# Linear attention ahead of two expert layers: 24 tiles pipelined two ahead, prefix sums in rounded parts, inputs in long rows

## Chip, cores and metric

One core of one Trainium2 chip runs the program. The metric is the time of one execution on the device in microseconds; the kernel before took 841.25 us (median of 3 runs, 837.5 to 843.47).

## The reference

```python
def _attn_ref(q, k, v, a_re, a_im):                # q: 4 batches, 8 heads, 768 positions, 48 wide
    mag = np.sqrt(a_re * a_re + a_im * a_im)
    scale = np.minimum(mag, 0.999) / (mag + 1e-06)
    a_re_n, a_im_n = (a_re * scale, a_im * scale)
    for t in range(S):
        S_re, S_im = ar * S_re - ai * S_im + k[t] v[t]^T, ar * S_im + ai * S_re
        y[:, :, t] = np.einsum('bhd,bhde->bhe', q[:, :, t], S_re)
    return y
```

The result, 3072 rows of 384, goes through two mixture-of-experts layers with 8 experts each (384 to 1024 to 384). The first sends each row to the expert whose normalised embedding is nearest; the second sends a row to the best of 8 gate scores if its skip score is positive, and adds the result to the row.

## The kernel before, in words

**Tiles.** The 768 positions are 6 chunks (c) of 128, one position a partition, for 4 batches (b): 24 tiles of 128 x 384 (8 heads of 48). Tile n is 4c + b. Within a tile the recurrence is attention with a causal mask, and a state `st` per batch passes from chunk to chunk.

**Preparation of a chunk**, all four batches at once (128 x 1536). The decay is taken as a logarithm of the size and an angle: squares (`squares`, GpSimd from chunk 2 on, ScalarE for chunks 0 and 1), logarithms and exponentials (`logs_a` to `logs_c`), the quotient (`slopes`, VectorE), the bound of the size (`slopes`, `clipped`), the arctangent (`angles`). PE sums both over positions with triangular matrices, one tile of 384 columns at a time (`sums`, lines 1445 to 1449: the log sum, the angle sum, and `last_row`, which carries over the last chunk's angle). ScalarE makes `ep` and `em`, exp of plus and minus the log sum (`decays`); VectorE brings the angle to turns (`turns`) and takes its absolute value (`turns_abs`, `ab`); ScalarE makes sine and cosine (`sines`, `cs`). GpSimd multiplies q and k by `ep` and `em` (`decayed`), and VectorE multiplies those by `cs` (`products`), which gives `qcs` and `kcs`.

**A tile on PE:** `transposes` of `qcs` and `kcs` through two banks (ScalarE copies them out as `qT` and `kT`), `scores` (VectorE masks them into `pm`), `state`, `outputs` (`pm` with v, and `qT` with `st`), and `router_row`, which turns the output back to positions and adds the 8 expert scores. VectorE's `rows` copies that into `ysb`, and line 1012 is its last instruction; `decay` renews `st`. `pick`, `rank` and `place` find each row's place in the expert's list, and GpSimd writes it by an indirect DMA (`send`).

**Order.** Each engine runs a list that is written out by hand, with semaphores between them. On PE and ScalarE chunks 1 to 4 are a loop. PE's list for tile n is: scores of n, router row of n-1, transposes of n+1, sums of the next chunk, state, sums, outputs of n. The products of a whole next chunk stand in VectorE's list from the row of tile 4c+1 on. The squares of chunk c+2 stand in GpSimd's list in the middle of chunk c.

**Inputs.** Each of q, k, v, a_re and a_im is [batch, head, position, 48] in memory, so one DMA of a tile moves pieces of 192 bytes.

**Experts.** After the last row, tables are computed from the counts, then for each layer slots of up to 512 gathered rows are multiplied by an expert's weights, which are split in a rounded part (fp32r) and a remainder (`w1h`, `w1l`; `xh`, `xl`): each product is three fp32r matmuls. This part has the same instructions after the change.

Of the kernel before, what the change touches and what calls it, by code (L numbers as in the profile page):

```python
# [22 lines left out]
P = 128  # L23
# [4 lines left out]
def build(nc, q, k, v, a_re, a_im, emb, tau, w1_a, w2_a, w_skip, w_gate, w1_b, w2_b, out):  # L28
    B, H, S, D = q.shape
    C = S // P  # L30
    HD = H * D
# [9 lines left out]
    CAP = 4096  # L41
# [20 lines left out]
    with keep:  # L62
# [13 lines left out]
        tri_half = const("tri_half", [P, P])  # L76
        tri_turn = const("tri_turn", [P, P])
# [93 lines left out]
        pm = t_("pm", [P, H * P])  # L171
# [43 lines left out]
        s_zero = sem("s_zero")  # L215
# [40 lines left out]
        s_sum1 = sem("s_sum1")  # L256
# [22 lines left out]
        s_first = sem("s_first")  # L279
# [31 lines left out]
        s_lgb = sem("s_lgb")  # L311
# [46 lines left out]
        def _(sp):  # L358
            def load_a(c):
                for b in range(B):  # L360
                    sp.dma_start(ar[:, b * HD:(b + 1) * HD].rearrange("p (h d) -> p h d", h=H), dram_tile(a_re, b, c)).then_inc(s_a_in, 16)
                    sp.dma_start(ai[:, b * HD:(b + 1) * HD].rearrange("p (h d) -> p h d", h=H), dram_tile(a_im, b, c)).then_inc(s_a_in, 16)

            def load_qk(c):
                for b in range(B):
                    sp.dma_start(qe[:, b * HD:(b + 1) * HD].rearrange("p (h d) -> p h d", h=H), dram_tile(q, b, c)).then_inc(s_qk_in, 16)
                    sp.dma_start(ke[:, b * HD:(b + 1) * HD].rearrange("p (h d) -> p h d", h=H), dram_tile(k, b, c)).then_inc(s_qk_in, 16)

            def load_v(b, c):
                sp.dma_start(vt[:, b, :].rearrange("p (h d) -> p h d", h=H), dram_tile(v, b, c)).then_inc(s_v_in[b], 16)  # L370
# [1372 lines left out]
```

## Time and profile before

| | us |
|---|---|
| timed runs, median of 3 | 841.25 (837.5 to 843.47) |
| the profiled execution | 833.39 |
| its span, first to last instruction | 831.7 |
| mean granted TensorE clock | 0.927 |
| PE busy, whole span | 672.9 (81%) |
| VectorE (DVE) busy | 511.0 (61%) |
| ScalarE (ACT) busy | 405.5 (49%) |
| GpSimd (POOL) busy | 320.5 (39%) |

### The profile page before, as it was taken

The page shows a single profiled execution, that of the slowest core. Times are in us where ns is not written, and L with a number is a line of the kernel's source. Part 1 is how long each engine was busy: PE and PEld are TensorE (multiplying, and loading weights), DVE is VectorE, ACT ScalarE, POOL GpSimd, SP SyncE. Part 2 cuts the span into 40 slices and gives each one's busy share as a digit, 9 for nine tenths or more (in the row PEclk, how much of TensorE's full clock was granted, in tenths as well). Part 3 has the DMA queues.
Part 4 walks back from the last instruction along what each step waited for, and adds up shares of the span by engine and source line. Part 5 has one row for each costly group of instructions (what it writes and reads, how often), then busy time and mean ns, then how long its engine had stood idle before and what let it go on. Part 6 is the DMA issues. An engine that isn't in the chain of part 4 may idle for free.

```text
span 831.7 us, 15914 instructions
## 1 busy us (share of the span) xinstructions
PE 672.9 (81%) x4794; PEld 611.1 (73%) x4794; DVE 511.0 (61%) x1155; ACT 405.5 (49%) x724; POOL 320.5 (39%) x328
## 2 busy tenths in 40 slices
PE   0549889797887999539999999999992289999993
PEld 0247767766777788438889999998892289999993
DVE  4464876858868585626457466566544367677770
ACT  5585564745747454116345354455341145455550
POOL 4302617326173223241353643642314404355531
PEclk9959889898998999859999999999997599999997
DMA  8936164281732435042352432543420336546530
GB/s 175 294 52 131 21 124 88 43 169 39 134 77 40 95 60 183 22 135 89 125 182 83 155 113 97 199 129 115 155 76 32 100 106 212 179 159 232 193 105 19
DMA packets 183385, 98.47 MB, mean 118 GB/s; under 512 B 151714, under 2 KB 171692, under 8 KB 183340
## 3 DMA queue, kind: packets, MB, share of 16 engines
q1 hardware_dynamic: 172844, 83.08, 36.6%
q0 software_dynamic: 10496, 14.84, 5.6%
q8 instruction: 21, 0.34, 0.2%
q14 instruction: 24, 0.20, 0.1%
HBM read 86.79 MB, written 22.09 MB: 131 GB/s over the span
## 4 chain that ended last, share of the span: by engine, by line
PE 71%; issue 7%; ACT 7%; DVE 6%; SPq 4%; DMA 2%; POOL 1%; POOLq 0%; DVEq 0%; ACTq 0%
PE bank L1616 8%; PE bank L1618 7%; PE bank L1617 7%; PE bank L1633 5%; PE bank L1634 4%; PE bank L1635 4%; PE bank L1461 4%; PE bank L1472 4%; PE bank L1501 3%; PE bank L1485 3%; PE bank L1649 3%; PE bank L1651 3%; PE bank L1650 3%; PE bank L1502 3%; PE bank L1663 3%
## 5 line engine op out<-in xcount | busy, mean ns | idle before, releaser
L1616 PE MATMUL bank<-xh,w1h 128*128 128x256 f32 (+3 forms) x384 | 125.0, 326 | 12.1 <-issue 5.8
L844 ACT ACTIVATE hh<-bank 128x256 fp32r<-128x256 f32 (+3 forms) x128 | 57.7, 451 | 136.9 <-PE bank L1618 136.9
L1617 PE MATMUL bank<-xh,w1l 128*128 128x256 f32 (+3 forms) x384 | 123.3, 321 | 0.0
L1618 PE MATMUL bank<-xl,w1h 128*128 128x256 f32 (+3 forms) x384 | 123.2, 321 | 0.0
L1237 DVE SCALAR_TENSOR_TENSOR hl<-bank,hh 128x256 fp32r<-128x256 f32 (+3 forms) x128 | 64.9, 507 | 61.8 <-ACT hh L844 54.5
L608 POOL DMA_INDIRECT out<-yg,idx_o x64 | 67.2, 1050 | 77.3 <-DVE yg L1298 45.6
L1616 PEld LDWEIGHTS bank<-xh,w1h 128*128 128x128 f32 x384 | 74.6, 194 | 17.2 <-issue 16.1
L1617 PEld LDWEIGHTS bank<-xh,w1l 128*128 128x128 f32 x384 | 74.7, 194 | 1.0
L1618 PEld LDWEIGHTS bank<-xl,w1h 128*128 128x128 f32 x384 | 74.4, 194 | 1.1
L520 POOL TENSOR_TENSOR qe<-qe,ep 128x384 f32<-128x384 f32 x24 | 25.4, 1060 | 126.5 <-DMA ke<-in_k 67.1
L1071 DVE TENSOR_TENSOR w2l<-raw,w2h 128x384 fp32r<-128x384 f32 x128 | 71.1, 555 | 0.0
L1633 PE MATMUL bank<-hh,w2h 128*128 128x384 f32 (+1 forms) x192 | 67.6, 352 | 1.7 <-issue 1.2
L618 POOL DMA_INDIRECT list<-pay,idx_b x32 | 37.0, 1156 | 82.4 <-DVE pay L1366 60.7
L1635 PE MATMUL bank<-hl,w2h 128*128 128x384 f32 (+1 forms) x192 | 66.5, 346 | 0.0
L1634 PE MATMUL bank<-hh,w2l 128*128 128x384 f32 (+1 forms) x192 | 66.4, 346 | 0.0
L765 ACT ACTIVATE w2h<-raw 128x384 fp32r<-128x384 f32 x128 | 66.2, 517 | 0.0
L537 POOL DMA_INDIRECT list<-token,idx_a x24 | 30.4, 1268 | 88.8 <-DVE idx_a L1053 73.7
L1071 DVE TENSOR_TENSOR w1l<-raw,w1h 128x1024 fp32r<-128x1024 f32 x48 | 58.4, 1224 | 9.8 <-issue 7.2
L590 POOL DMA_INDIRECT xg<-out,idx_g x32 | 34.1, 1066 | 73.4 <-DVE yg L1320 53.0
L1501 PE MATMUL bank<-pm,vt 128*48 128x128 f32 x384 | 44.9, 303 | 17.3 <-DVE ysb L1012 17.3
L1604 PE MATMUL bank<-ident,xg 128*128 128x128 f32 (+1 forms) x132 | 21.3, 293 | 46.3 <-DMA xg<-out,idx_g 25.9
L836 ACT ACTIVATE xh<-bank 128x256 fp32r<-128x256 f32 (+3 forms) x48 | 19.5, 451 | 69.6 <-PE bank L1604 68.3
(232 smaller groups left out, 1692.0 us busy)
## 6 DMA issues: line engine op xcount, KB each, us to landing
raw<-in_moe_w SPq DMA_DIRECT2D x32, 1536.0 KB, 6.9
x_a<-ysb SPq DMA_DIRECT2D x24, 196.0 KB, 2.9
ar<-in_a_re SPq DMA_DIRECT2D x24, 192.0 KB, 3.8
ai<-in_a_im SPq DMA_DIRECT2D x24, 192.0 KB, 3.8
qe<-in_q SPq DMA_DIRECT2D x24, 192.0 KB, 3.8
ke<-in_k SPq DMA_DIRECT2D x24, 192.0 KB, 3.7
vt<-in_v SPq DMA_DIRECT2D x24, 192.0 KB, 3.5
list<-nobody SPq DMA_DIRECT2D x2, 2048.0 KB, 10.2
```

Of the source, the lines that this page charges most:

```text
L608: g.indirect_dma_start(out, bass.IndirectOffsetOnAxis(idx_o[:, par, j:j + 1], 0), yg[:, par, j, :], None, bounds_check=N - 1, oob_is_err=F ...
L765: return a.activation(hi[:, at], raw[:, at], ACT.Copy)
L844: a.activation(hh[:, f, 0:n], U[f % 3][:, 0:n], ACT.Relu).then_inc(s_hh[m], 1)
L1071: return d.tensor_tensor(lo[:, at], raw[:, at], hi[:, at].bitcast(F32), ALU.subtract)
L1237: d.scalar_tensor_tensor(out=hl[:, f, 0:n], in0=U[f % 3][:, 0:n], scalar=0.0, in1=hh[:, f, 0:n].bitcast(F32), op0=ALU.max, op1=ALU.subtrac ...
L1501: t.matmul(to, vt[:, b, h * D:(h + 1) * D], pm[:, h * P:(h + 1) * P], start=True, stop=False)
L1616: t.matmul(U[f % 3][:, 0:n], wh, xh[:, k_, 0:n], start=k_ == 0, stop=False)
L1617: t.matmul(U[f % 3][:, 0:n], wl, xh[:, k_, 0:n], start=False, stop=False)
L1618: i = t.matmul(U[f % 3][:, 0:n], wh, xl[:, k_, 0:n], start=False, stop=k_ == KC - 1)
L1633: t.matmul(DN[d_ % 2][:, 0:n], wh, hh[:, f, 0:n], start=f == 0, stop=False)
L1634: t.matmul(DN[d_ % 2][:, 0:n], wl, hh[:, f, 0:n], start=False, stop=False)
L1635: i = t.matmul(DN[d_ % 2][:, 0:n], wh, hl[:, f, 0:n], start=False, stop=f == FC - 1)
```

## The change

**Inputs.** The host lays q and k, and a_re and a_im, side by side as [batch, position, 2, 384], and v as [batch, position, 384]. One DMA now brings both of a pair for a tile, in rows of 3072 bytes. The lists hold 3072 entries an expert instead of 4096. The list of layer 1 is cleared later (after step 3), and the a of chunk 1 is asked for before the lists are cleared.

**Chunk 0 in halves.** All preparation passes over chunk 0 are cut in two pairs of batches; its prefix sums go to different banks (`sum_bank`, `turn_bank`), VectorE takes one of the two squares, sines are made one tile at a time, and no instruction for chunk 1 stands before the sines of chunk 0 on ScalarE.

**Pipeline over tiles.** Every engine runs `step(n)` for 24 tiles, with no loop instructions. In step n PE does scores(n+1), state(n), outputs(n), transposes(n+2) with queries and keys apart, router_row(n). VectorE does rows(n-1), masked(n+1), state_sum(n), products(n+2), decay(n). `pm` and `qcs` are held twice. The preparation of later chunks is threaded in at given steps; the absolute value is now taken a tile at a time into `cs` (`folds`).

**Sums from parts.** From chunk 2 on the log and the angle are split: `lh`, `ah` (ScalarE copies, rounded to fp32r), `ll` (GpSimd) and `al` (VectorE) are the remainders. Each sum is then two fp32r matmuls with `half_r` and `one_r`. `last_row` stays f32.

```diff
@@ sync @@
+                    sp.dma_start(a_t[:, b, :, :], a[b, c * P:(c + 1) * P, :, :]).then_inc(s_a_in[b // 2], 16)
+                sp.dma_start(qk_t[:, b, :, :], qk[b, c * P:(c + 1) * P, :, :]).then_inc(s_qk_in[b], 16)
+                sp.dma_start(vt[:, b, :], v[b, c * P:(c + 1) * P, :]).then_inc(s_v_in[b], 16)
...
@@ gpsimd @@
+            def log_low(c):
+                pool.wait_ge(s_lh, c - 1)
+                for b in range(B):
+                    g.tensor_tensor(ll[:, b, :], lm[:, b, :], lh[:, b, :].bitcast(F32), ALU.subtract).then_inc(s_ll, 1)
...
+            for c in range(2, C - 1):
+                if c + 2 < C:
+                    square_im(c + 2)
+                decayed(c + 1, 0)
+                decayed(c + 1, 1)
+                if c + 2 < C:
+                    square_sum(c + 2)
+                sends(c - 1, 2)
+                decayed(c + 1, 2)
+                decayed(c + 1, 3)
+                sends(c, 0)
+                if c + 3 < C:
+                    square_re(c + 3)
+                if c + 2 < C:
+                    log_low(c + 2)
...
@@ scalar @@
+                if second and b == 1:
+                    decays(c + 1, 2)
+                outputs_T(n)
+                queries(n + 2)
...
+                if second and b == 0:
+                    decays(c + 1, 0)
+                if second and b == 1:
+                    decays(c + 1, 3)
+                if c and third and b == 2:
+                    angles(c + 2)
+                if c and third and b == 3:
+                    inverse_size(c + 2)
+                keys(n + 2)
...
+                if second and b == 0:
+                    decays(c + 1, 1)
+                    if third:
+                        log_re(c + 2)
+                        inverse_re(c + 2)
+                if c and c + 1 < C and b == 1:
+                    trig_table()
+                    sines(c + 1, 0, 2)
+                    sines(c + 1, 2, 4)
+                if c and third and b == 2:
+                    angle_high(c + 2)
+                    exp_table()
+                    log_size(c + 2)
+                if c and third and b == 3:
+                    log_extra(c + 2)
+                    log_high(c + 2)
...
@@ vector @@
+                if n:
+                    rows(n - 1)
...
+                if second and b == 1:
+                    turns(c + 1, 1)
+                    folds(c + 1, 1)
...
+                if b == 0 and c and c + 1 < C:
+                    bounded(c + 1)
+                    clipped(c + 1)
+                masked(n + 1)
...
+                if b == 0 and c:
+                    pick(c - 1, 2)
+                state_sum(n)
...
+                products(n + 2)
...
+                decay(n)
...
+                if c and third and b == 1:
+                    slopes(c + 2)
+                if c and third and b == 3:
+                    angle_low(c + 2)
...
@@ tensor @@
-                t.matmul(PL[:, 0:HD], tri_half[:, :], lm[:, b * HD:(b + 1) * HD], start=True, stop=True).then_inc(s_L, 1)
+                    t.matmul(to, half_r[:, :], lh[:, b, :], start=True, stop=False)
+                    pe.wait_ge(s_ll, B * (c - 2) + b + 1)
+                    t.matmul(to, half_r[:, :], ll[:, b, :], start=False, stop=True).then_inc(s_L, 1)
...
```

The first place is VectorE at the first tile of chunk 3, before: `pm` are the masks, `kk` and `turn` the turns of chunk 4, `st_sum` and `st` the state. The clip of the log (L961) and two products stand ahead of the masks.

```order
L961 SCALAR_TENSOR_TENSOR lm<-le,lm 128x1536 [waits s_mn,s_le]
L988 TENSOR_TENSOR qcs<-qe,cs 128x768 [waits s_Y,s_qe]
L988 TENSOR_TENSOR kcs<-ke,cs 128x768
L998 TENSOR_TENSOR pm<-bank,causal 128x512 [waits s_Y,s_score]
L998 TENSOR_TENSOR pm<-bank,causal 128x512 [waits s_score]
L971 TENSOR_SCALAR kk<-bank 128x384 [waits s_turn,s_TH,s_cs]
L973 TENSOR_TENSOR turn<-bank,kk 128x384 [waits s_kk]
L1061 TENSOR_TENSOR st_sum<-bank,st 96x384 [waits s_state,s_U]
L1066 TENSOR_TENSOR st<-st_sum,dec 96x384 [waits s_dec,s_Y,s_added]
```

The same place after, which is step 12: bound and clip of the log, masks, the pick, the state sum, and then the products, which are those of tile 14.

```order
L1124 TENSOR_SCALAR lm<-lm 128x1536 [waits s_rm]
L1131 SCALAR_TENSOR_TENSOR lm<-le,lm 128x1536 [waits s_mn,s_le]
L1181 TENSOR_TENSOR pm<-bank,causal 128x512 [waits s_Y,s_score]
L1181 TENSOR_TENSOR pm<-bank,causal 128x512 [waits s_score]
L1211 TENSOR_TENSOR sum_a<-sum_a,two_a 128x8 [waits s_two,s_rank]
...
L1221 TENSOR_TENSOR oh_a<-ch_p,first_of 128x16 [waits s_ch]
L1244 TENSOR_TENSOR st_sum<-bank,st 96x384 [waits s_state,s_U]
L1170 TENSOR_TENSOR qcs<-qk_t,cs 128x768 [waits s_T,s_U,s_qe,s_cs]
L1170 TENSOR_TENSOR kcs<-qk_t,cs 128x768
L1253 TENSOR_TENSOR st<-st_sum,dec 96x384 [waits s_dec,s_Y,s_added]
```

What moved: the products were at the end of the chunk before, ahead of this tile's masks; now a pair stands in each tile, behind masks, pick and state sum, for the tile two ahead.

The second place is PE at the same tile, before, where the banks are the numbered ones of the program (0 and 1 transposes, 2 and 3 scores, 4 log sum, 5 angle sum, 6 outputs, 7 state).

```order
L1472 MATMUL bank2<-qT,kT 128x128 [waits s_pm]
...
L1461 MATMUL bank0<-ident,qcs 96x128 [waits s_Tout]
...
L1461 MATMUL bank1<-ident,kcs 96x128 [waits s_Tout]
...
L1445 MATMUL bank4<-lm,tri_half 128x384 [waits s_exp]
L1448 MATMUL bank5<-an,tri_turn 128x384 [waits s_turn]
L1449 MATMUL bank5<-turn,last_row 128x384
...
L1485 MATMUL bank7<-vt,kcs 96x48 [waits s_v_in0]
...
L1501 MATMUL bank6<-pm,vt 48x128 [waits s_pm]
```

And PE after, in the first step of a middle chunk.

```order
L1697 MATMUL bank2<-qT,kT 128x128 [waits s_pm,s_Tout]
...
L1714 MATMUL bank7<-vt,kcs 96x48 [waits s_v_in0,s_added]
...
L1731 MATMUL bank6<-pm,vt 48x128 [waits s_pm,s_state,s_y]
...
L1683 MATMUL bank0<-ident,qcs 96x128 [waits s_Tout,s_prod]
...
L1636 MATMUL bank4<-lh,half_r 128x384 [waits s_lh,s_exp]
L1638 MATMUL bank4<-ll,half_r 128x384 [waits s_ll]
L1660 MATMUL bank5<-ah,one_r 128x384 [waits s_ah,s_turn]
L1662 MATMUL bank5<-al,one_r 128x384 [waits s_al]
L1663 MATMUL bank5<-turn,last_row 128x384
L1683 MATMUL bank0<-ident,kcs 96x128 [waits s_Tout,s_prod]
...
L1739 MATMUL bank6<-aug,yT 128x120 [waits s_yt]
```

What moved: the transposes went from before state and outputs to behind them, for tile n+2 instead of n+1, and their wait (s_prod) is now for products made in the same step; the sums of one tile stand between queries and keys.

## Rows read from the trace of the kernel before

**Rows 1.** Stretches between tile rows: PE, PEld, DVE, ACT, POOL busy; clock; DMA.
```profile
0.00:71.40 71.40, 29.95 (x162) 21.93 (x163) 36.49 (x45) 46.33 (x50) 18.16 (x60) 0.88 0.79 175
71.40:114.10 42.70, 34.76 (x272) 29.36 (x271) 28.26 (x46) 24.66 (x32) 21.45 (x13) 0.88 0.25 47
114.10:166.30 52.20, 44.62 (x401) 38.19 (x401) 38.30 (x69) 31.30 (x41) 22.45 (x15) 0.93 0.46 91
166.30:217.60 51.30, 42.91 (x386) 36.50 (x385) 38.04 (x70) 30.44 (x40) 22.44 (x15) 0.93 0.47 93
217.60:269.00 51.40, 42.44 (x384) 36.01 (x383) 38.29 (x69) 30.20 (x41) 22.43 (x15) 0.93 0.46 93
269.00:312.10 43.10, 39.78 (x375) 33.43 (x374) 30.12 (x68) 22.35 (x35) 12.05 (x12) 1.00 0.38 75
312.10:344.50 32.40, 30.17 (x338) 27.90 (x336) 17.07 (x52) 11.96 (x20) 8.13 (x6) 1.00 0.36 124
```

**Rows 2.** Timeline of chunk 2, 187 to 201 us: GpSimd, VectorE and PE.
```profile
187.10 0.43 PE L1501 MATMUL bank<-pm,vt 128*48 128x128 f32 x4
...
188.59 2.74 POOL L528 TENSOR_TENSOR sqi<-ai 128x1536 f32<-128x1536 f32 x1
...
189.22 2.54 DVE L1066 TENSOR_TENSOR st<-st_sum,dec 96x384 f32<-96x384 f32 x1 [3.45 <-PE bank L1502]
...
191.41 3.63 POOL L530 TENSOR_TENSOR m<-m,sqi 128x1536 f32<-128x1536 f32 x1
...
191.76 3.31 DVE L1046 TENSOR_TENSOR two_a<-oh_a 128x8 bf16<-128x8 bf16 x1
...
200.96 0.67 PE L1501 MATMUL bank<-pm,vt 128*48 128x128 f32 x4 [5.41 <-DVE ysb L1012]
```

**Rows 3.** The stretch behind that wait, columns as in rows 1.
```profile
200.90:206.80 5.90, 5.84 (x48) 5.46 (x49) 4.16 (x10) 3.08 (x4) 0.84 (x1) 0.61 0.17 37
```

**Rows 4.** Timeline of the start: ScalarE and PE.
```profile
12.44 1.47 ACT L675 ACTIVATE m<-ar 128x1536 f32<-128x1536 f32 x1
...
24.18 1.28 ACT L700 ACT_TABLE_LOAD   x1
...
27.38 1.65 PE L1445 MATMUL bank<-lm,tri_half 128*128 128x384 f32 x2 [15.06 <-DVE lm L961]
...
41.87 1.48 ACT L675 ACTIVATE m<-ar 128x1536 f32<-128x1536 f32 x1 [3.14 <-DMA ai<-in_a_im]
...
50.90 1.94 PE L1461 MATMUL bank<-ident,qcs 128*96 128x128 f32 x8 [10.92 <-DVE kcs L988]
```

**Rows 5.** Timeline of chunk 2, 205 to 219 us: VectorE.
```profile
205.22 0.95 DVE L988 TENSOR_TENSOR qcs<-qe,cs 128x768 f32<-128x768 f32 x1
...
206.96 1.28 DVE L998 TENSOR_TENSOR pm<-bank,causal 128x512 f32<-128x512 f32 x2
...
215.99 0.95 DVE L956 TENSOR_SCALAR lm<-lm 128x1536 f32<-128x1536 f32 x1
...
218.51 1.75 DVE L961 SCALAR_TENSOR_TENSOR lm<-le,lm 128x1536 f32<-128x1536 f32 x1
```

**Rows 6.** Timeline of PE: f32 sums (185 us), fp32r matmuls of the experts (376 us).
```profile
185.01 0.88 PE L1445 MATMUL bank<-lm,tri_half 128*128 128x384 f32 x2
...
186.37 0.81 PE L1449 MATMUL bank<-turn,last_row 128*128 128x384 f32 x2
...
376.50 0.33 PE L1617 MATMUL bank<-xh,w1l 128*128 128x384 f32 x1
376.68 0.33 PE L1618 MATMUL bank<-xl,w1h 128*128 128x384 f32 x1
```

**Rows 7.** Timeline of PE in the last chunk: transposes, state, scores of a tile.
```profile
321.39 1.04 PE L1461 MATMUL bank<-ident,qcs 128*96 128x128 f32 x8
...
323.74 1.54 PE L1485 MATMUL bank<-vt,kcs 128*96 128x48 f32 x16
...
327.14 2.05 PE L1472 MATMUL bank<-qT,kT 96*128 96x128 f32 x16
```

More of the change, by code:

```diff
@@ L805, in _ @@
[L805 to L818 removed]
+                sines(0, b, b + 1)
@@ L820, in _ @@
+            for n in range(NT):
+                step(n)
             for m in range(2):
@@ L967, in turns @@
+            def turns(c, b):
                 n = B * c + b
+                if c:
+                    dve.wait_ge(s_cs, B * (c - 1) + b + 1)
                 dve.wait_ge(s_TH, n + 1)
-                if not (first and b == 0):
+                if n:
                     dve.wait_ge(s_turn, n)
-                d.tensor_scalar(kk[:, :], PTH[:, 0:HD], ROUND, -ROUND, ALU.add, ALU.add).then_inc(s_kk, 1)
+                angle = turn_bank(c, b)[:, 0:HD]
+                d.tensor_scalar(kk[:, :], angle, ROUND, -ROUND, ALU.add, ALU.add).then_inc(s_kk, 1)
@@ L1107, in _ @@
-            modulus(0)
             slopes(0)
+            bounded(0)
             clipped(0)
             for b in range(B):
-                turns(0, b, True)
-            turns_abs(0)
-            modulus(1)
-            for b in range(B):
-                products(0, b, True)
-            masked(0, 0)
-            slopes(1)
-            decay(0, 0)
-            masked(0, 1)
-            clipped(1)
-            rows(0, 0)
-            turns(1, 0)
-            decay(0, 1)
-            turns(1, 1)
@@ L1126, in _ @@
-            turns(1, 2)
-            masked(0, 2)
-            rows(0, 1)
-            pick(0, 0)
-            turns(1, 3)
-            turns_abs(1)
-            decay(0, 2)
-            masked(0, 3)
-            rows(0, 2)
-            products(1, 0)
-            decay(0, 3)
-            place(0, 0)
-            products(1, 1)
-            products(1, 2)
-            slopes(2)
-            rows(0, 3)
-            pick(0, 2)
-            clipped(2)
-            products(1, 3)
-            for c in range(1, C - 2):
-                chunk(c)
@@ L1147, in _ @@
-            chunk(C - 2, two=False)
-            for b in range(B):
-                masked(C - 1, b)
-                if b:
-                    rows(C - 1, b - 1)
-                if b == 2:
-                    pick(C - 1, 0)
-                decay(C - 1, b)
-                if b == 1:
-                    place(C - 2, 2)
-                if b == 3:
-                    place(C - 1, 0)
-            rows(C - 1, B - 1)
+                turns(0, b)
+                folds(0, b)
+            products(0)
@@ L1160, in _ @@
+            for n in range(NT):
+                step(n)
+            rows(NT - 1)
             pick(C - 1, 2)
@@ L1571, in _ @@
-            transposes(1, 0)
-            router_row(0, B - 1)
-            with pe.Fori(1, C - 1) as c:
-                chunk(c)
-            chunk(C - 1, one=False)
+                angle_sum(0, b)
+            for n in range(2):
+                transposes(n, 0)
+                transposes(n, 1)
+            scores(0)
+            for n in range(NT):
+                step(n)
             rank(C - 1, 2, True)
```

1002 lines of the change are left out of this document (572 added, 430 removed).

## Prediction, made before the result was known

> **What bounds the kernel now.** I read the stretches between tile rows first, then the timeline of one chunk, then the start. Attention writes 24 tile rows (reduction L1012 ends each); the stretches of [rows 1] are cut at the rows of tile 0, of tile 3, 7, 11, 15, 19 and 23. The reader should see three regimes. Up to 71.4 us only one tile is out. A middle chunk takes 51.3 to 52.2 us with PE busy 42.4 to 44.6 of them: PE leads, but it is not full. The last chunk, which has no next chunk to prepare, takes 32.4 us with PE busy 30.2: 8.1 us a tile, PE bound. All that follows 344.5 us, 487.2 us of the span, is mixture-of-experts code whose instructions the change leaves as they are.
>
> Why is PE not full in a middle chunk? [Rows 2] show one case, which comes back once a chunk. GpSimd squares 1536 columns from 188.59 to 191.33 and adds them from 191.41 to 195.04. VectorE's `st` update, started at 189.22, takes 2.54 us and ends only at 191.76; the 8-column `two_a` takes 3.31 and ends at 195.07. VectorE, five us late, delivers the masked scores and the row late, and PE stands 5.41 us before `outputs` at 200.96. Then PE's granted clock is 0.61 over the next 5.9 us [rows 3], near the 1.2 GHz level: its matmuls there take 0.67 us a group instead of 0.43, and the stall costs about 2.5 us more.
>
> The Trainium skill says in "SBUF — State Buffer", section "SBUF: two separate sides", that VectorE instructions with two SBUF inputs and GpSimd instructions exclude each other for a whole instruction; the two stretched rows agree.
>
> **The start (before 71.4 us).** Before, ScalarE's first square starts at 12.44, the first prefix sum on PE at 27.38; all four tiles' sums share one bank; at 41.87 ScalarE squares chunk 1, waiting 3.14 us for its DMA, ahead of chunk 0's sines; the first transposes start at 50.90 [rows 4]. After, work is in halves, DMAs bring 3072-byte rows in 4 issues instead of 8, VectorE takes one square, and no square of chunk 1 stands ahead. ScalarE can start near 7 (after its table load, 1.28) and makes 12 half passes of 1.47/2 = 0.74: 9 us, with a wait for the second half about 18. VectorE has the embedding work in between and ends the first clipped half near 19. Four prefix sums go to four banks and four pairs of exponentials follow at 1 us each: 24. A table load, the arctangent: 26.5. Then VectorE's turn (two 384-column passes, about 0.55 each by [rows 5]: 1.28 for two of 512) and fold (1.75/4 = 0.45) four times: 6.6, and to 34. Products (0.95 each) to 36: first transposes near 36.5, 14.4 us earlier. But two tiles, four groups of 1.94 at the low clock plus copies, are now transposed ahead of the first scores: 9 us, scores 3.5 at that clock, and step 0 (scores 1, state, outputs, transposes of tile 2, router, row) about 9: 58. **Gain 13.4.** By nearest rows it lies between 7 (the a tiles land no sooner, and VectorE's embedding work is late) and 17.
>
> **The rest of chunks 0 and 1 (42.7 and 52.2 us).** The chain for the next chunk (logs, sums, exponentials, arctangents, turns, sines) is still threaded through tiles 1 to 5 in order: step 2's angle sums wait for ScalarE's arctangent, the products of tile 4 for the sines, scores 4 for keys copied behind the second sine pass. I add these to 11, 18 and 12.5 us for tiles 1 to 3 (41.5) and 51 for chunk 1. **Gain 1.2 and 1.2**, each -5 to +6.
>
> **A middle chunk (51.3 and 51.4 us, chunks 2 and 3).**
> *PE's share.* A prefix sum in f32 over 384 columns is two records, 0.68 us by the step 185.01 to 186.37 for two of them; in rounded form one instruction follows the next after 0.18 [rows 6]. Log and angle now take 4 x 0.18 = 0.7 in place of 1.36: 0.65 less a tile, 2.6 a chunk. The `last_row` matmul stays f32. The other work of a tile stays as it is, 8.1 with its short waits: scores about 2, state 1.4, outputs 1.8 (eight groups that overlap by half), two groups of transposes and the router 0.9 each [rows 7].
> *Added.* Two ScalarE copies of 1536 columns (1.47 each), against two table loads fewer (1.28 each): even, and ScalarE is busy 30 of 51. One VectorE pass of 1536 with two SBUF inputs (`al`, 1.75 as L961): VectorE goes from 38 to 40 busy. GpSimd gets four subtractions of 384 columns, each a quarter of 2.74 to 3.63 [rows 2] and a little more, about 1 us: from 22.4 to 26.4.
> *Steps between router rows, four a chunk (b = 0 to 3).* VectorE now makes products for tile n+2 between `state` and `outputs`, so PE's transposes wait for it when it is late. b=0: row 0.75, bound 0.95, clip 1.75, masks 1.28, pick 1.1, state sum 0.55, products 1.85 [rows 5] make 8.4 with latency before the transposes; PE then adds 0.9 + 1.4 (sums) + 0.9 + 0.9: 12.6. PE's own way to the transposes is 2 + 1.4 + 1.8 = 5.2, so it stands 3 us. b=1 has three turns and `slopes`: VectorE is busy 13.6, PE 12; 12.5. b=2 and b=3: PE bound, 9.2 each. Floor **43.5**.
> *What comes on top.* ScalarE ends `log_extra` after the keys, so the clip of b=0 starts about 0.9 late; ScalarE's `log_high` is queued in front of `outputs_T`, and behind it GpSimd's `ll` falls together with the products of b=0; `square_sum` falls on those of b=1, `square_re` on b=3. Each meeting costs up to what [rows 2] show (2.0 and 3.2 for one instruction). With 15.5, 13.7, 10.5 and 11.5 the chunk is 51.2, and with one more spell of low clock [rows 3] 53.7. I take **49**, inside these ends and nearer to the upper, as the locks are seen in each chunk of before: **gain 4.7 in two chunks**; 43.5 gives 15.7, 53.7 gives -4.7.
>
> The Trainium skill's rule of the shared ports speaks against this change: it moves two-input VectorE products from a stretch in which GpSimd idles into one where it works. By the rule alone every meeting is paid in full, and the chunk would be the 51.2 above; without it 43.5.
>
> **Chunks 4 and 5 (43.1 and 32.4 us).** Before, chunk 4 is short since only sums, turns and sines are left; after, its b=0 still has bound, clip, pick and products ahead of the transposes. Floor 42, top 47, taken 44.5: **-1.4**. Chunk 5: tiles 20 and 21 at 9.2, then 7 and 5.1, as no transposes are left: 30.5, **+1.9**.
>
> **Hidden at nothing.** The loads in long rows within the steady chunks: GpSimd waited for them, but nobody waited for GpSimd's products then. The shorter lists (3072 entries an expert) only lighten the start. The w1/w2 loads come earlier; the first gather, which waits for the last row and the lists, sets that moment.
>
> **Sum.** 13.4 + 1.2 + 1.2 + 4.7 - 1.4 + 1.9 = 21.0. The profiled execution took 833.4 (span 831.7): 812.4. The median of the timed runs is 841.25, 0.9% above the profiled one, so the forecast for the median is 841.25 - 21 = 820.
>
> **Rivals.**
> *A, the meetings don't happen and the pipeline reaches its floor.* Chunks 2 and 3 at 43.5, chunk 4 at 42, chunks 0 and 1 4 us better each: 13.4 + 5.2 + 5.2 + 15.7 + 1.1 + 1.9 = 42.5: 799. For it: VectorE and GpSimd two-input work in a chunk, about 17 and 22 us, fits into 45. Against: [rows 2].
> *B, only the start gains, and less.* The start at 65 because of the landing and the embedding work, chunks 1 to 4 even: 6.4 + 1.9 = 8: 833. For it: 27.38 to 50.90 is a serial chain, and only part of it is overlapped now.
> *C, the clock.* In b=0 PE stands before the transposes for as long as VectorE is late. The floor gives 3 us, the upper case 5 or more, which is the stall after which [rows 3] show 0.61. If each chunk from 1 on has two such spells, and the wait reaches 8 us because `ll` and products alternate, a middle chunk costs 57: chunks 1 to 4 lose 5 + 6 + 6 + 6 = 23, against 15 from start and end: 8 slower, 849. It decides from a middle chunk over 55 us. For it: PEclk is 0.93 in each middle chunk already. Against: the two matching waits of before (5.4 us at b=2) go, so a spell replaces a spell.
> The Trainium skill, "TensorE: Matmul & The Clock Gate", section "HAM oscillation — how this bites in real kernels", has PE come back from idle time at half its clock in each round of a loop; the row at 0.61 agrees, and for C it would hold in each chunk.
>
> **How the numbers follow.** Forecast 0.6, A 0.2, B 0.15, C 0.03, other 0.02. Range 799 to 834: from A's time to just past B's. About 1% (8.4 us) is what a measurement here tells from no change: faster by more is anything under 832.8, which is the forecast, A and two thirds of B: 0.91; within 1% 0.07; slower 0.02.
>
> **What would show it.** Tile 0's row near 58 us and tile 3's near 100. Steady chunks of 46 to 51.5 us; PE idle before `qcs` transposes, released by VectorE's products, largest at b=0 and 3 to 5 us there; products that take 1.5 us or more where GpSimd runs; no 5.4 us wait at `outputs`. The last row near 323, and 487 us after it. I am wrong in mechanism if the wait for the products is under 1 us everywhere, if the start gains under 8 us, or if the part after the last row moves by more than 5 us.

## The result, and the profile after

The change made the kernel slower: 854.41 us (849.74 to 859.97, 4 runs) against 839.38 (832.56 to 843.47, 4 runs), ratio 1.019 [1.0096, 1.0284]. The forecast was 820, range 799 to 834. The profiled execution of after has a span of 852.0, so 20.3 more than before, and the stretches below add up to just that.

The stretches of after, cut at the rows of tiles 0, 3, 7, 11, 15, 19 and 23 as in [rows 1] (the columns are the same: length, then busy us of PE, PEld, DVE, ACT, POOL, then clock, DMA share, GB/s):

```profile
0.00:59.74 59.74, 27.71 (x164) 20.03 (x165) 36.88 (x50) 39.83 (x60) 28.93 (x62) 0.86 0.45 141
59.74:110.64 50.90, 38.27 (x287) 31.57 (x285) 32.00 (x52) 23.56 (x35) 20.62 (x13) 0.87 0.33 101
110.64:174.33 63.69, 45.32 (x384) 40.23 (x384) 47.06 (x74) 38.29 (x48) 31.64 (x20) 0.84 0.32 101
174.33:227.67 53.34, 42.80 (x384) 38.17 (x384) 42.46 (x74) 31.60 (x43) 33.01 (x20) 0.90 0.31 91
227.67:280.50 52.83, 43.17 (x384) 38.59 (x384) 42.11 (x73) 31.60 (x43) 27.49 (x19) 0.90 0.23 62
280.50:324.40 43.90, 38.96 (x392) 35.56 (x393) 34.68 (x71) 22.93 (x36) 20.51 (x16) 1.00 0.34 95
324.40:356.10 31.70, 26.65 (x307) 24.62 (x305) 17.22 (x51) 9.54 (x15) 9.20 (x6) 1.00 0.26 93
356.10:852.00 495.90, 412.11 (x2490) 391.60 (x2490) 284.88 (x745) 208.02 (x469) 191.32 (x192) 0.92 0.38 126
```

Line by line against [rows 1]: the start gains 11.7, and it is the only large gain. The rest of chunk 0 loses 8.2, chunk 1 11.5, chunks 2 and 3 2.0 and 1.4, chunk 4 0.8, chunk 5 gains 0.7. The last line, whose instructions are the same as before, loses 8.7. Three places show where the time went.

**A middle chunk, b=0.** VectorE and PE behind the row of tile 11, the place of the order listings:

```profile
227.59 1.42 DVE L1124 TENSOR_SCALAR lm<-lm 128x1536 f32<-128x1536 f32 x1
229.14 1.76 DVE L1131 SCALAR_TENSOR_TENSOR lm<-le,lm 128x1536 f32<-128x1536 f32 x1
230.82 1.28 DVE L1181 TENSOR_TENSOR pm<-bank,causal 128x512 f32<-128x512 f32 x2
...
233.94 0.94 DVE L1170 TENSOR_TENSOR qcs<-qk_t,cs 128x768 f32<-128x768 f32 x1
234.81 0.94 DVE L1170 TENSOR_TENSOR kcs<-qk_t,cs 128x768 f32<-128x768 f32 x1
```

```profile
232.59 0.43 PE L1732 MATMUL bank<-qT,st 96*48 96x128 f32 x4
235.81 1.47 PE L1683 MATMUL bank<-ident,qcs 128*96 128x128 f32 x8 [2.80 <-DVE kcs L1170]
...
238.36 1.48 PE L1663 MATMUL bank<-turn,last_row 128*128 128x384 f32 x2
```

PE has its outputs done at 233 and stands 2.80 us for products that VectorE makes behind bound, clip, masks and pick. The products take 0.94 each: no meeting with GpSimd is in the products themselves. The same wait ends at 252.92 (2.69) and at 265.54 (1.65), and behind each of the three the clock is low:

```profile
235.70:240.70 5.00, 4.89 (x24) 4.13 (x25) 2.05 (x4) 2.42 (x5) 5.00 (x4) 0.66 0.00 0
252.70:257.70 5.00, 4.78 (x23) 4.01 (x24) 4.42 (x7) 2.31 (x5) 2.98 (x3) 0.66 0.01 2
266.70:270.70 4.00, 3.68 (x21) 3.59 (x22) 0.12 (x2) 4.00 (x6) 0.92 (x1) 0.57 0.00 0
```

So in chunk 3 one wait of 5.4 us with one spell of low clock [rows 2, 3] became three waits of 1.7 to 2.8 with three spells. A wait and a spell don't always go together, though. In chunk 2 the waits are 2.80, 2.14 and 2.47, and behind the second, the wait that ends at 200.63, the clock stays full:

```profile
200.60:206.00 5.40, 5.37 (x42) 5.02 (x43) 5.26 (x8) 4.29 (x8) 2.80 (x3) 1.00 0.01 2
```

The `last_row` sum of chunk 3 takes 1.48 in a spell and 0.81 outside [rows 6]. From row to row the four steps of chunk 3 take 14.9, 18.5, 10.2 and 9.2 us (16.0, 17.9, 9.7 and 9.7 in chunk 2): the longest is b=1, in which VectorE is busy 17.2 of 18.5 us (16.9 of 17.9).

**Chunk 1, step 5.** VectorE, GpSimd and PE:

```profile
135.17 7.44 DVE L1170 TENSOR_TENSOR kcs<-qk_t,cs 128x768 f32<-128x768 f32 x1
...
135.26 1.00 POOL L550 TENSOR_TENSOR qk_t<-qk_t,ep 128x384 f32<-128x384 f32 x1
...
138.11 0.98 POOL L551 TENSOR_TENSOR qk_t<-qk_t,em 128x384 f32<-128x384 f32 x1
...
139.06 2.74 POOL L563 TENSOR_TENSOR le<-a_t 128x1536 f32<-128x1536 f32 x1
...
141.94 3.98 POOL L568 TENSOR_TENSOR m<-m,le 128x1536 f32<-128x1536 f32 x1
...
142.54 3.79 DVE L1253 TENSOR_TENSOR st<-st_sum,dec 96x384 f32<-96x384 f32 x1
...
142.67 1.94 PE L1683 MATMUL bank<-ident,qcs 128*96 128x128 f32 x8 [8.19 <-DVE kcs L1170]
```

A 0.95 us product lasts until GpSimd has done its four decay products and a square, 7.44 us in all; PE stands 8.19.

**The experts.** Two matmuls of after stand behind idle time in which PE waited for nothing that the profile shows ("issue"). They come 48 and 346 us behind the last row:

```profile
404.39 0.68 PE L1869 MATMUL bank<-hh,w2h 128*128 128x384 f32 x1 [2.87 <-issue]
...
701.69 0.57 PE L1852 MATMUL bank<-xh,w1h 128*128 128x256 f32 x1 [3.73 <-issue]
```

Before has no such stand above 1.5 us. Behind the first, matmuls of 384 columns take 0.52 us instead of 0.33 for 6 us, at the low clock. The queue that loads code (packets, MB, share), on the page of after and then on that of before:

```profile
q8 instruction: 31, 0.51, 0.3%
```

```profile
q8 instruction: 21, 0.34, 0.2%
```

The program is longer, since 24 steps are written out where before has loops.

### The profile page after: what moved, and what is told of

Read it like the earlier page. It is cut to its first block, busy times and chain, and to the rows that moved or that the text cites. A ratio compares the mean times of both kernels' runs of the same rounds, so it can differ in the third digit from the quotient of the medians.

```text
span 852.0 us, 15924 instructions
## 1 busy us (share of the span) xinstructions
PE 675.0 (79%) x4786; PEld 620.4 (73%) x4786; DVE 537.3 (63%) x1182; ACT 405.4 (48%) x744; POOL 362.7 (43%) x346
## 4 chain that ended last, share of the span: by engine, by line
PE 54%; issue 5%; DVE 2%; DMA 2%; POOL 1%; ACT 1%; POOLq 0%; DVEq 0%; ACTq 0%
PE bank L1852 8%; PE bank L1853 7%; PE bank L1854 7%; PE bank L1869 5%; PE bank L1871 4%; PE bank L1870 4%; PE bank L1885 3%; PE bank L1887 3%; PE bank L1886 3%; PE bank L1899 3%; PE bank L1840 2%; PE bank L1683 1%; PE bank L1697 1%; PE bank L1714 1%; PE bank L1739 1%
## 5 line engine op out<-in xcount | busy, mean ns | idle before, releaser
L1683 PE MATMUL bank<-ident,qcs 128*96 128x128 f32 x192 | 32.7, 324 | 53.1 <-DVE kcs L1170 53.0
L678 POOL DMA_INDIRECT list<-pay,idx_b x32 | 36.6, 1145 | 83.4 <-DVE pay L1552 52.8
L1683 PEld LDWEIGHTS bank<-ident,qcs 128*96 128x96 f32 x192 | 24.4, 147 | 61.3 <-DVE kcs L1170 59.6
L1840 PE MATMUL bank<-ident,xg 128*128 128x128 f32 (+1 forms) x132 | 21.1, 294 | 44.7 <-DMA xg<-out,idx_g 26.2
L581 POOL DMA_INDIRECT list<-token,idx_a x24 | 27.3, 1139 | 68.1 <-DVE idx_a L1236 53.7
L1697 PE MATMUL bank<-qT,kT 96*128 96x128 f32 x384 | 50.7, 287 | 5.7 <-ACT kT L826 5.7
```

Of the source, the lines that this page charges most:

```text
L1683: i = t.transpose(T[j % 2][0:D2, (h % 4) * P:(h % 4 + 1) * P], src.rearrange("p a d -> p (a d)"), ident[:, :])
L1697: i = t.matmul(PT[j][:, (h % 4) * P:(h % 4 + 1) * P], kT[:, n % 2, h * P:(h + 1) * P], qT[:, n % 2, h * P:(h + 1) * P], start=True, stop=True)
```

## Experiments

In what follows a stand is idle time of PE, and a meeting is a VectorE instruction that runs longer beside one of GpSimd.

Theory W: PE waits for products that VectorE makes too late in its step, and the clock falls behind each wait. Theory P: the meetings of VectorE and GpSimd set the pace. Theory S: the split's passes cost more than the shorter sums give. Theory F: the experts' stands come of where their code lies. Theory G, its rival: they come of the shorter lists or of where the data lies.

All stretches in us, cut as above; a median is of that kernel's timed runs. In brackets behind a ratio stands its 95% interval.

| | start | chunk 0 | 1 | 2 | 3 | 4 | 5 | behind last row | median |
|---|---|---|---|---|---|---|---|---|---|
| before | 71.4 | 42.7 | 52.2 | 51.3 | 51.4 | 43.1 | 32.4 | 487.2 | 839.4 |
| after | 59.7 | 50.9 | 63.7 | 53.3 | 52.8 | 43.9 | 31.7 | 495.9 | 854.4 |
| e1 | 59.9 | 47.9 | 56.1 | 50.9 | 50.4 | 47.1 | 31.2 | 495.3 | 841.2 |
| e2 | 60.4 | 49.2 | 63.4 | 51.4 | 50.1 | 46.1 | 31.7 | 495.9 | 851.1 |
| e3 | 60.5 | 51.3 | 62.3 | 54.0 | 53.2 | 47.7 | 35.3 | 494.7 | 860.0 |
| e4 | 60.3 | 47.4 | 48.2 | 51.5 | 51.8 | 45.4 | 31.2 | 495.6 | 834.5 |
| e5 | 61.1 | 50.8 | 62.7 | 52.8 | 51.1 | 43.9 | 31.7 | 493.9 | 852.8 |
| e6 (before) | 71.1 | 43.7 | 53.1 | 50.3 | 51.0 | 42.9 | 32.4 | 516.0 | 858.9 |
| e7 | 60.4 | 49.1 | 50.0 | 46.7 | 45.1 | 47.2 | 34.1 | 494.8 | 829.0 |
| e8 | 61.3 | 46.4 | 46.0 | 43.3 | 43.3 | 42.4 | 33.7 | 490.6 | 806.8 |
| e9 | 60.1 | 46.4 | 48.5 | 48.2 | 48.1 | 47.2 | 33.7 | 490.7 | 824.0 |
| e10 (before) | 70.6 | 39.4 | 47.8 | 45.7 | 45.7 | 43.0 | 32.4 | 506.3 | 831.3 |
| e11 | 60.4 | 51.8 | 55.5 | 49.8 | 48.1 | 46.0 | 32.2 | 501.2 | 846.9 |

Beside e1 to e4 the kernel before took 834.8, beside e5 to e7 834.3, beside e8 and e9 834.7; e10 and e11 ran on a chip on which it took 847.7, so they are read by ratio and by the stretches of attention. No profile of before was taken on that chip: how much of the 506.3 and 501.2 behind the last row is the chip and how much the kernel stays open.

**e1, products first.**

```diff
+                if n != 2:
+                    products(n + 2)
                 if b == 3:
                     place(c, 0)
...
-                products(n + 2)
+                if n == 2:
+                    products(n + 2)
```

> VectorE's step order only: products(n+2) right behind rows(n-1), ahead of bound, clip, masks, pick and state sum (in step 2 it stays where it was). Theory W (PE waits for the products, 2.8, 2.7 and 1.7 us in chunk 3, and each wait is followed by low clock, 10 us of it a chunk): chunks 2 and 3 go from 53.3 and 52.8 to 46 to 49, the waits before the qcs transposes fall under 1 us, the total falls by 10 to 18 us from 854. Rival P (the meetings with GpSimd set the pace): products meet GpSimd elsewhere, chunks stay within 1.5 us of 53.

841.23, ratio to before 1.0087 [1.0045, 1.0129], 13 less than after. The waits before the `qcs` transposes are gone, but chunks 2 and 3 fall only to 50.9 and 50.4, short of 46 to 49. In them VectorE is now busy 46.0 and 44.7 instead of 42.5 and 42.1, with the same instructions: more of it is spent in meetings with GpSimd. In b=1 the products meet it, and PE stands in a new place instead, before `state`, once in each of the two chunks:

```profile
232.15 1.74 DVE L1170 TENSOR_TENSOR kcs<-qk_t,cs 128x768 f32<-128x768 f32 x1
...
234.08 2.77 PE L1717 MATMUL bank<-vt,kcs 128*96 128x48 f32 x16 [3.88 <-issue]
```

Both theories hold a part.

**e2, squares on ScalarE.**

```diff
+            def squares(c):
+                a_.activation(m2[:, :, :], a_t[:, :, 0, :], ACT.Square).then_inc(s_sq, 1)
+                a_.activation(le[:, :, :], a_t[:, :, 1, :], ACT.Square).then_inc(s_sq, 1)
...
                     if third:
+                        squares(c + 2)
                         log_re(c + 2)
```

> The two squares of chunks 2 to 5 go from GpSimd to ScalarE (2 x 1.47 us a chunk there, 5.5 us less on GpSimd); the sum stays on GpSimd. Theory P: the stretched VectorE instructions (8 to 12 us over a chunk) mostly go; chunk 1 falls from 63.7 by 7 or more (its kcs product of 7.4 us becomes 1), chunks 2 and 3 by 3; total 12 us less. Theory W: chunk 1 falls as under P, since its 7.4 us stands right before a PE wait, but chunks 2 and 3 move by under 1.5 us; total 7 us less. If ScalarE is the tighter one: chunks 2 and 3 slower by 1 to 3.

851.12, ratio 1.0188 [1.0119, 1.0258]. Chunks 2 and 3 fall by 1.9 and 2.8, nearer to P (3) than to W (under 1.5); chunk 1 does not move (63.4), against both theories. Its long product is back at 0.94, but the fold in front of it now takes the hit from GpSimd's sum, which stayed there, and ScalarE's squares delay the exponentials:

```profile
132.86 0.69 PE L1639 MATMUL bank<-lh,half_r 128*128 128x384 f32 x1 [4.02 <-ACT em L811]
...
136.91 3.43 POOL L568 TENSOR_TENSOR m<-m,le 128x1536 f32<-128x1536 f32 x1
...
137.07 3.68 DVE L1158 SCALAR_TENSOR_TENSOR cs<-turn 128x384 f32<-128x384 f32 x1
```

**e3, f32 sums from two buffers.**

```diff
-                    t.matmul(to, half_r[:, :], lh[:, b, :], start=True, stop=False)
-                    t.matmul(to, half_r[:, :], ll[:, b, :], start=False, stop=True).then_inc(s_L, 1)
+                t.matmul(to, tri_half[:, :], LM[c % 2][:, b, :], start=True, stop=True).then_inc(s_L, 1)
```

> The rounded parts undone: sums in f32 from two buffers of log and angle, so no lh, ah, al, ll. Theory S (the split's passes cost more than the shorter sums give: 3 us ScalarE, 1.75 VectorE, 4 to 6 GpSimd a chunk): chunks 2 and 3 fall by 1 to 4, total 5 to 12 less. Rival (PE bound): each of chunks 2 to 4 rises by 2 to 2.6, total 6 to 8 more.

860.04, ratio 1.0286 [1.0216, 1.0356], 5.6 more than after; theory S falls. Chunks 2 and 3 rise by 0.7 and 0.4 only, chunks 4 and 5 by 3.8 and 3.6. Not all of this is the sums: chunk 5 has none, and in both chunks the mean clock is lower than in after (0.96 and 0.86 for 1.00). What the parts save on PE shows between kernels whose chunk 4 runs at a clock of 1.00 throughout: PE is busy 38.96 us there in after, and 41.52 in e4 with f32 sums.

**e4, all three:** the edits of e1, e2 and e3 in one kernel.

> The three edits together. If the causes are the three named and add up: chunks 2 and 3 near 44 to 46, chunk 1 near 50, total near 820 to 828, faster than before (839) and after. If PE in f32 is then the bound: 46 to 48 a chunk and 828 to 836.

834.53, ratio 1.0008 [0.9972, 1.0045]: level with before. The total lies in the range of the second case (828 to 836), but chunks 2 and 3, at 51.5 and 51.8, lie outside both forecasts; chunk 1 is down to 48.2. One meeting does it, once a chunk in b=1; VectorE, GpSimd and PE of e4:

```profile
221.91 3.80 POOL L571 TENSOR_TENSOR m<-m,le 128x1536 f32<-128x1536 f32 x1 [0.78 <-ACT le L743]
...
222.35 4.18 DVE L1136 TENSOR_TENSOR kcs<-qk_t,cs 128x768 f32<-128x768 f32 x1
226.45 0.16 DVE L1194 TENSOR_TENSOR at_f<-bank,oh_a 128x16 f32<-128x16 f32 x1
...
226.72 1.49 PE L1667 MATMUL bank<-vt,kcs 128*96 128x48 f32 x8 [5.42 <-issue]
```

PE waits before `state` for VectorE's `place` (`at_f`), which stands behind the long product; the profile calls the wait "issue", and that it is this one is read from the order of times.

**e7, the sum on VectorE too.**

```diff
-                if c + 2 < C:
-                    square_sum(c + 2)
...
                 masked(n + 1)
+                if c and third and b == 1:
+                    square_sum(c + 2)
```

> The run with all three edits (834.5; chunks 1, 2, 3 at 48.2, 51.5, 51.8), and the sum of the squares of chunks 2 to 5 on VectorE (1.75 us) behind the masks of b=1 instead of on GpSimd. Theory P (one meeting left: kcs takes 4.2 us beside GpSimd's sum, PE stands 5.4 us before state, low clock for 6 us): chunks 2 and 3 fall to 43 to 46, total to 815 to 822. Rival W (the chain of sums, turns and sines sets b=1 anyway): 49 to 52 a chunk, total 830 to 836.

829.02, ratio 0.9943 [0.9921, 0.9966]. Against e4 chunks 2 and 3 fall by 4.8 and 6.7 to 46.7 and 45.1 (43 to 46 forecast): theory P for the chunks. The total is 7 short of its forecast, since chunks 0, 1, 4 and 5 rose by 1.7 to 2.9 each. In chunks 4 and 5 the mean clock is lower than in e4 (0.96 and 0.90 for 1.00 in both), with no wait of PE above 0.9 us in chunk 5; the same holds for chunk 5 of e3, e8 and e9.

**e5 and e6, where the experts' code stands.** The edit is the same in both, with 376 waits in after and 648 in before:

```diff
             t.matmul(PC, minus[:, :], sum_a[:, :], start=False, stop=True).then_inc(s_count, 1)
+            for _ in range(376):
+                pe.wait_ge(s_exp, B * C)
```

> After, with 376 waits that are already met (12,032 bytes of code) on PE behind the counts, where it stands 18 us for the first gather anyway. That moves the experts' code to where it stands in before, counted modulo 32 KB. Theory F (8.6 us of the loss lie in the experts: PE stands 2.9 us at 48 us and 3.7 at 345 us behind the last row for code that is still being fetched, and the clock drops behind both): the part behind the last row falls from 495.9 to 487 to 489, the two stands to under 1.7 us, the total by 8. Rival G (it comes of the lists with 3072 entries, or of the data's addresses): 495 to 496 as before, stands in place.

> Before, with 648 such waits (20,736 bytes) at the same place, which gives its experts' code the place that it has in after, modulo 32 KB. Theory F: the part behind the last row rises from 487.3 to 494 to 496, with stands of 2.5 to 4 us near 48 and 345 us. Rival G: 487 to 488, or up to 491 if the waits themselves take longer than the idle time that hides them.

e5 as a whole is 852.81, ratio 1.0232 [1.0196, 1.0267]: the part behind the last row falls to 493.9 only, for 487 to 489 forecast. The waits themselves take longer than the idle time that was to hide them. So the experts are counted from their first transposes, one row each of before, after, e5 and e6:

```profile
364.55 1.32 PE L1604 MATMUL bank<-ident,xg 128*128 128x128 f32 x5 [18.65 <-DMA xg<-x_a,idx_g]
```

```profile
376.01 1.32 PE L1840 MATMUL bank<-ident,xg 128*128 128x128 f32 x5 [18.52 <-DMA xg<-x_a,idx_g]
```

```profile
378.55 1.75 PE L1842 MATMUL bank<-ident,xg 128*128 128x128 f32 x7 [23.15 <-issue]
```

```profile
383.87 1.53 PE L1606 MATMUL bank<-ident,xg 128*128 128x128 f32 x6 [37.89 <-issue]
...
711.27 0.57 PE L1618 MATMUL bank<-xh,w1h 128*128 128x256 f32 x1 [3.87 <-issue]
```

From there to the end before takes 831.7 - 364.6 = 467.1 and after 476.0. Shifted, after takes 847.9 - 378.6 = 469.3, and before 860.5 - 383.9 = 476.6, with a stand of 3.87 us (last row) at the place where after has 3.73. Theory F stands in both directions, and G falls: before has its old lists. The edit adds waits in both kernels, and one becomes faster and the other slower behind them, so it is not the waits themselves. What is left is the position of unchanged code. The other kernels agree. The late stand (3.1 to 4.0 us) is in all of e1 to e4 and e7, which take 475.0 to 476.2 from the first transposes, and in none of e5, e8, e9 and e11, which hold the 376 waits. The first stand (2.87 us) becomes 2.12 in e5 and 1.92 in e6, so that one the position explains only in part. e6 as a whole is 858.93, ratio 1.0293 [1.0264, 1.0321], 19.2 us of it the waits: its first transposes come 39.3 us behind the last row instead of 20.1.

**e8, the best version:** e7, and three edits.

```diff
+            for _ in range(120):
+                pe.wait_ge(s_tri, 3)
...
+                if b == 3:
+                    place(c, 0)
+                if b == 1 and c:
+                    place(c - 1, 2)
                 if n != 2:
                     products(n + 2)
...
                 if n == 2:
-                    sines(1, 0, 2)
+                    sines(1, 0, 1)
```

> The last run (829.0) and three edits: place ahead of the products in b=1 and 3 (PE stood 2.2 us before state for it); in step 2 the sines of tile 4 alone, its products ahead of turn (1,1), sines of tiles 6 and 7 behind the keys (step 2 took 18 us, 1.8 to 3 us of it waits for these); 12,032 bytes of met waits on PE, 120 at the start and 256 behind the counts, both where PE stands anyway. Theories F and W: chunks 2 and 3 at 43.5 to 45.5, chunk 0 behind tile 0 at 44 to 47, the part behind the last row at 487 to 489; total 812 to 818. If the shift brings nothing: 819 to 825.

806.77 (801.83 to 808.93), ratio to before 0.9662 [0.9626, 0.9697], better than forecast. Chunk 0 is at 46.4; the part behind the last row, 490.6, falls by 4.2 against e7, and misses the 487 to 489. The two middle chunks:

```profile
153.59:196.88 43.29, 40.54 (x384) 34.98 (x384) 35.44 (x74) 31.17 (x43) 13.36 (x12) 1.00 0.39 112
196.88:240.16 43.28, 40.70 (x384) 34.98 (x384) 35.89 (x74) 31.16 (x43) 13.40 (x12) 1.00 0.29 76
```

PE is busy 40.6 of 43.3 at the full clock, without the rounded parts. The experts take 806.8 - 335.8 = 471.0 from their first transposes. Chunk 5 is 33.7 for 31.7 in after: in its last tile the clock falls to half, though PE's waits there (0.69 and 0.85 us) are those of after, where it stays at 1.00. A row of PE and the stretch behind it:

```profile
306.79 2.30 PE L1674 MATMUL bank<-vt,kcs 128*96 128x48 f32 x16 [0.85 <-issue]
...
308.00:316.00 8.00, 6.76 (x47) 5.93 (x46) 1.62 (x4) 0.60 (x1) 1.94 (x2) 0.50 0.03 5
```

**e9, the rounded parts in the best version:** the parts as in the change, but `ll` on VectorE, and in b=0 clip and bound ahead of the products.

```diff
+                if second and b == 0:
+                    log_low(c + 1)
...
-            log_low(2)
```

> The same with the rounded parts of the change, but the low part of the log made on VectorE, in four pieces (4 x 0.45 to 0.55 us) behind clip and products in b=0, so GpSimd has only decays and sends. If PE is the bound once the meetings are gone, chunks 2 to 4 fall by 2 to 2.6 against the run beside it, total 806 to 812. If the chain (clip, high part, low part, first sum) or VectorE (40 us busy) is the bound, the chunks are the same or up to 3 slower.

823.97, ratio 0.9874 [0.9836, 0.9913], 17 us more than e8; the miss is large. PE of e9 in b=0:

```profile
212.61 0.33 PE L1650 MATMUL bank<-ll,half_r 128*128 128x384 f32 x1
215.71 0.44 PE L1672 MATMUL bank<-ah,one_r 128*128 128x384 f32 x1 [2.76 <-DVE turn L1139]
```

VectorE's turn, which frees the bank of the angle sum, now stands behind clip, products, `ll` (1.96), masks and pick. PE stands 2.8 us in b=0 of each middle chunk, and the clock falls (0.89 in chunk 3): chunks 2 and 3 are 4.9 and 4.8 longer than in e8, where the shorter sums would save about 2 us each.

**e10, before without GpSimd's squares:** squares on ScalarE, their sum (`modulus`) on VectorE.

```diff
                 decays(c + 1, 2)
+                if two:
+                    squares(c + 2)
...
                 decay(c, 1)
+                if two:
+                    modulus(c + 2)
```

> Before, with the squares of chunks 2 to 5 on ScalarE (into its idle 6 us behind decays 2) and their sum on VectorE, nothing else. Theory P (the meetings cause the 5.4 us wait and the low clock of b=2 in before too): that wait falls under 2 us, chunks 1 to 4 of before fall from 52.2, 51.3, 51.4 to 45 to 48, total from 834.5 to 818 to 824: about half of what the best version gains would need no new pipeline. Rival (one tile ahead, the chain of sums, turns and sines sets b=1 and 2 anyway): 50 to 52 a chunk, total 830 to 836.

831.32 beside 847.74 for before on the same chip, ratio 0.9798 [0.9742, 0.9855]. The wait of 5.41 us [rows 2], 5.75 in chunk 3 of before, is 1.42 in chunk 3 of e10:

```profile
203.63:249.32 45.69, 40.91 (x386) 34.64 (x385) 34.12 (x71) 33.12 (x43) 13.73 (x12) 1.00 0.52 104
234.55 0.43 PE L1505 MATMUL bank<-pm,vt 128*48 128x128 f32 x4 [1.42 <-DVE ysb L1013]
```

Chunks 2 and 3 fall from 51.3 and 51.4 to 45.7, and the clock is 1.00. That is 2.0% of the 3.4% that e8 gains, without a new pipeline, and theory P for the kernel before. In attention alone it is 19.8 us (last row at 324.7 for 344.5) of e8's 28.3.

**e11, the best version with the change's late products** (and without the edits in step 2).

```diff
-                if n != 2:
-                    products(n + 2)
...
                 state_sum(n)
+                products(n + 2)
```

> The best version (806.8; chunks 2 and 3 at 43.3) with VectorE's products back behind bound, clip, masks, pick and state sum, as the change has them, and without the edits in step 2: squares off GpSimd, f32 sums, code shift stay. Theory W (products that are made in the step that transposes them make PE stand, and the clock fall, without any meeting too): chunks 2 and 3 at 48 to 51, waits of 2 to 3 us before the qcs transposes in b=0 and 1, total 824 to 834. Rival P (only the meetings count): 43.5 to 45, total 808 to 815.

Ratio to before 0.9988 [0.9956, 1.0021]. Chunks 2 and 3 are 49.8 and 48.1 instead of 43.3, though GpSimd meets hardly anything (POOL busy 14). The wait is the one of after:

```profile
225.07 1.08 PE L1640 MATMUL bank<-ident,qcs 128*96 128x128 f32 x8 [2.29 <-DVE kcs L1137]
```

Late products cost 6.5 and 4.8 us a chunk, without meetings. That is the first half of theory W. The second half, that the clock falls behind each wait, is not seen here. Chunk 3 of e11:

```profile
217.43:265.53 48.10, 40.81 (x384) 34.98 (x384) 35.78 (x74) 31.15 (x43) 14.54 (x12) 1.00 0.26 68
```

PE is busy as long as in e8 (40.7), at the full clock: all of the 4.8 us is idle time. The total of 846.86 lies outside its range on account of the chip; by ratio it would be 0.9988 x 834.7 = 834, its upper end.

## Why the prediction was wrong

A gain of 21.0 was forecast, and the profiled execution lost 20.3. Of the 41.3 us between them chunk 1 holds 12.7, chunk 0 9.4, the part behind the last row 8.7, the two middle chunks 8.2, the start 1.7 and chunk 5 1.2; chunk 4 came out 0.6 better.

- **Start.** 13.4 forecast, 11.7 measured; tile 0's row at 59.7 for 58. Two errors offset each other, so the number is in part luck: the first transposes start at 41.6 and not at 36.5 (one product took 4.17 us), and from them to the row it is 18.2 us for 21.5.
- **Rest of chunks 0 and 1.** This step failed: a gain of 1.2 each was forecast, from a sum of guessed steps (11, 18, 12.5; then 51), and 8.2 and 11.5 were lost. The steps took 14.1, 21.4 and 15.5. The reason, read from the rows, is in the change itself: the chain for the next chunk must end one tile earlier, since products are needed two tiles ahead, and it does not start earlier. ScalarE and PE of after in step 2:

```profile
76.01 1.48 ACT L790 ACTIVATE an<-an 128x1536 f32<-128x1536 f32 x1
86.52 0.84 ACT L818 ACTIVATE cs<-turn 128x768 f32<-128x768 f32 x1 [9.03 <-DVE cs L1155]
90.10 1.30 PE L1683 MATMUL bank<-ident,qcs 128*96 128x128 f32 x5 [3.47 <-DVE kcs L1170]
```

  From arctangent to sines it is 10.5 us, with masks and a fold of 2.32 us between, and tile 4's transposes end the chain. e8's edits in this step bring chunk 0 to 46.4, still 3.7 above before. In chunk 1 the forecast did not see the queue of GpSimd: it priced a meeting at one instruction (2.0 to 3.2 us), and step 5 met five in a row. With products first chunk 1 takes 56.1 (e1), and with squares on ScalarE and f32 sums as well 48.2 (e4).
- **Middle chunks, 49 forecast, 53.3 and 52.8 measured.** The mechanism was right: PE stands before the `qcs` transposes, largest in b=0 (2.80; 3 to 5 forecast), and no 5.4 us wait is left at `outputs`. The meetings were put in the wrong place: steady products take 0.94; the stretched ones are folds, `two_a`, `idx_a` and `st`. Two terms were mis-sized. One is step b=1: 12.5 in the floor, less than the 13.6 that the same sentence has VectorE busy, and 13.7 in the upper case. It took 18.5 and 17.9, and VectorE was busy 17.2 and 16.9. The clock does not explain this, as in chunk 2 it was 1.00 in this step. The other is the clock in the other steps, which the floor left out: rival C had it ("each chunk from 1 on has two such spells"), at a chance of 0.03 and an argument ("a spell replaces a spell") that the three rows at 0.57 to 0.66 refute for chunk 3. Its price (57 a chunk) was too high, its side was right. That its total of 849 lies near the 854 is luck: it lost nothing in chunk 0 and behind the last row, where 16.9 us went.
- **PE's share, 2.6 us a chunk from the rounded parts.** The size was right: 38.96 us of PE in chunk 4 for 41.52 (e4), both at the full clock. It was booked in full though PE was not full in a middle chunk, where e3 gives it 0.4 to 0.7 us, and e9 shows that the passes behind it can cost more.
- **The floor of 43.5** is real: e8 reaches 43.3, by another way than the change (f32 sums, early products, no squares on GpSimd).
- **Chunks 4 and 5:** -1.4 and +1.9 forecast, -0.8 and +0.7 measured.
- **Behind the last row:** "instructions unchanged" was taken for "time unchanged". It cost 8.7 us, the second loss by size.
- **By the forecast's own test** ("if the part after the last row moves by more than 5 us") it was wrong in mechanism too; the other two tests it passed (the wait is 2.80, the start gains 11.7).

The Trainium skill, "Runtime: NRT & Kernel Launch", section "Instruction fetch mechanics", has code loaded in blocks of 16 KiB and a taken branch out of the loaded window wait for a load. The experts branch by slot length, and the 31 packets with 0.51 MB on the page of the profile of after are 16 KB each, which agrees; e5 and e6 show that position decides, not that a load is what PE waits for. That remains open.

The Trainium skill's rule of the ports that VectorE and GpSimd share ("SBUF — State Buffer", section "SBUF: two separate sides") has the one that starts first hold them for a whole instruction. The trace agrees and goes further: VectorE did not get in between five instructions of GpSimd that followed each other at once (7.44 us for 0.95).

Also open: why the stand at 48 us moved by only a part in e5 and e6, what decides whether the clock falls behind a wait or in the last tile, and how much of the start's gain each of its edits brings; none was tried apart.

## What to carry to other kernels

When a pipeline is made deeper, ask for each engine what is queued ahead of the instruction that the bounding engine waits for: products moved to the front of VectorE's step were worth 4.8 and 6.5 us a chunk (e11 against e8), with no work removed. Take long work off GpSimd before the order is tuned at all, since the squares and their sum held VectorE and, through it, PE and its clock (5.7 us a chunk in the kernel before). Look up the granted clock behind each short wait of PE. Where it is low it has a price (5 us at 0.66, so 1.7 us, for each of the first two here), but it can't be taken for granted: it stayed at 1.00 behind 2.14 us in chunk 2 and throughout chunk 3 of e11. Compare the parts that were not edited, too.

## What was not expected of the hardware

- A 0.95 us VectorE product lasted 7.44 us beside five GpSimd instructions in a row.
- Waits of PE as short as 1.65 us were followed by 4 us at a granted clock of 0.57, near the 1.2 GHz level, after a stretch that already had two longer ones. A wait of 2.14 us in the same kernel and one of 2.29 in e11 were followed by 1.00, and the last tile of e8 ran at 0.50 behind waits of 0.69 and 0.85.
- Moving unchanged code by 648 waits (20,736 bytes) made the experts 9.5 us slower, moving it by 376 waits (12,032 bytes) in the longer program 6.7 us faster.
- A wait that is already met took about 60 ns on PE: 648 of them stand in 37.89 us without a matmul, 376 in 23.15.
